# Attention, gating and experts in one program: SBUF laid out by hand, and the experts' weight loads issued at other places

## The reference

```python
# attention: B,H,S,D = 4,8,1152,64
q_pool = q.reshape(B, H, S // 2, 2, D).mean(axis=3)
attn = softmax(q_pool @ k.T / sqrt(D))          # 576 x 1152 per head
x = (attn @ v)                                  # -> tokens: 2304 x 512
# soft mixture: 8 experts, 4 slots each
logits = x @ phi                                # 2304 x 32
slot_input = softmax(logits, axis=0).T @ x      # 32 x 512
for e in range(8):                              # w1: 512 x 1024, w2: 1024 x 512
    slot_out[e] = relu(slot_input[e] @ w1[e]) @ w2[e]
x = softmax(logits, axis=1) @ slot_out          # 2304 x 512
# MLP
h = x @ w_in                                    # 512 x 2048
out = (h - tanh(h)) @ w_out                     # 2048 x 512
```

## Time and profile before

| | us |
|---|---|
| median of 3 runs | 968.81 |
| the three runs | 969.33, 964.74, 968.81 |
| the profiled execution: its own time | 964.63 |
| the profiled execution: span from the first to the last instruction | 962.8 |

### The profile page before, as it was taken

How to read it: one execution, slowest core, us unless ns; L and a number is a source line. 1 busy time by engine, 2 the same in 40 slices (tenths; PEclk the granted TensorE clock), 3 DMA queues, 4 the chain that set the end, 5 groups by cost and what they waited for, 6 DMA issues and landing times. The chain is left out here.

```text
span 962.8 us, 16386 instructions
## 1 busy us (share of the span) xinstructions
PE 887.5 (92%) x5707; PEld 641.9 (67%) x5707; DVE 588.3 (61%) x1167; ACT 496.8 (52%) x711; POOL 313.6 (33%) x215
## 2 busy tenths in 40 slices
PE   3999999999999999999999998877568999999998
PEld 2776776776776776767767765553223788888886
DVE  3676676776766766776776765450004766666663
ACT  1655555555555555555555554221006766666662
POOL 3353244244235234234333300000005744444442
PEclk9999999999999999999999999988888999999999
DMA  4322202102112022022022000295995000000000
GB/s 123 105 61 75 73 4 74 52 22 74 36 37 74 11 63 74 0 74 74 0 74 74 1 25 1 91 347 226 398 406 193 12 23 22 22 22 22 22 22 33
DMA packets 48865, 75.50 MB, mean 78 GB/s; under 512 B 5056, under 2 KB 23488, under 8 KB 48320
## 3 DMA queue, kind: packets, MB, share of 16 engines
q1 hardware_dynamic: 48832, 75.06, 22.8%
HBM read 70.32 MB, written 4.72 MB: 78 GB/s over the span
## 5 line engine op out<-in xcount | busy, mean ns | idle before, releaser
L496 DVE TENSOR_REDUCE part_neg<-ps 128x1 f32<-128x512 f32 (+1 forms) x432 | 220.9, 548 | 7.0 <-PE ps L304 6.6
L320 PE MATMUL ps<-ident,prob 128*128 128x128 f32 x1296 | 205.3, 286 | 18.4 <-ACT prob L542 7.9
L320 PEld LDWEIGHTS ps<-ident,prob 128*128 128x128 f32 x1296 | 143.9, 141 | 105.2 <-DVE probT L415 38.7
L415 DVE COPY probT<-ps 128x512 f32<-128x512 f32 (+1 forms) x256 | 125.1, 489 | 143.4 <-PE ps L320 117.1
L542 ACT ACTIVATE prob<-ps,neg_max 128x1152 f32<-128x1152 f32 x144 | 175.6, 1219 | 58.7 <-DVE neg_max L500 58.2
L304 PE MATMUL ps<-kT,qT_hi 128*128 128x512 f32 (+1 forms) x480 | 176.3, 384 | 5.3 <-DVE qT_lo L205 5.2
L553 ACT ACTIVATE probT<-ps 128x512 f32<-128x512 f32 x144 | 86.2, 598 | 171.9 <-PE ps L320 170.1
L337 PE MATMUL ps<-probT,v_nat 128*64 128x256 f32 (+1 forms) x1152 | 167.5, 417 | 0.5 <-DVE probT L415 0.5
L304 PE MATMUL ps<-kT,qT_lo 128*128 128x512 f32 (+1 forms) x480 | 159.5, 356 | 0.0
L304 PEld LDWEIGHTS ps<-kT,qT_hi 128*128 128x128 f32 x480 | 95.4, 201 | 21.6 <-issue 11.2
L1005 PE MATMUL ps<-w_hi,g 128*128 128x512 f32 x320 | 102.6, 392 | 2.2 <-POOL g L1090 2.0
(11 more groups left out here) (146 smaller groups left out, 1093.2 us busy)
## 6 DMA issues: line engine op xcount, KB each, us to landing
ring<-in_moe_w SPq DMA_DIRECT2D x10, 2048.0 KB, 20.0
k_nat<-in_k SPq DMA_DIRECT2D x16, 576.0 KB, 4.0
v_nat<-in_v SPq DMA_DIRECT2D x16, 576.0 KB, 5.1
q_nat<-in_q SPq DMA_DIRECT2D x32, 256.0 KB, 4.5
w_first<-in_moe_w SPq DMA_DIRECT2D x4, 2048.0 KB, 13.9
out<-x SPq DMA_DIRECT2D x18, 256.0 KB, 2.0
x<-in_moe_w SPq DMA_DIRECT2D x2, 2048.0 KB, 11.4
x<-in_moe_w_in SPq DMA_DIRECT2D x1, 4096.0 KB, 29.5
```

Source lines behind the costliest of these rows:

```text
L320: last = nc.tensor.transpose(block_at(s, kt), src[:, kt * P:(kt + 1) * P], ident[:])
L415: return eng_copy(probT[g][:, k0:k1, h, col:col + P], src.rearrange("p (c q) -> p c q", c=n))
L496: nc.vector.reduce_max(part_neg[:, c:c + 1], slot_banks(s)[:, c, 0:(CHUNK[c][1] - CHUNK[c][0]) * P], AX.X, negate=True).then_inc(part_done, 1)
```

## The change

The tiles get fixed addresses from a table in place of the stacked allocations. The ring of five places becomes ten halves of 2 MB (16 KB per partition), `slot` 0 to 9; expert e uses halves 2(e mod 5) and 2(e mod 5) + 1. Halves 0 and 1 overlap no other tile. Halves 2 and 3 lie over the attention's k_nat, k_parts, q_nat, q_dup and q_raw, half 4 over kT and qT of the even pairs, half 5 over those of the odd pairs, half 6 over part of probT0, halves 7 and 8 over x, half 9 over the rest of probT0 and part of probT1, where the gating has xT and c_parts. Each expert has a semaphore for each of its matrices. What SP issues, and after what:

| where | before | now |
|---|---|---|
| pair 0 | w1[0] | w1[0], w2[0] |
| pair 15, ahead of its v | | w1[1], w2[1], after the last transposes and split of q and k |
| pair 15, behind its v | | w1[2], after pair 14's last scores |
| end of attention | | w2[2] after the last scores; w1[3] after the first half of the last pair's products with v |
| gating | w2[0], w1[1], w2[1], w1[2], w2[2], at once | w2[3], w1[4] after the slot inputs (L694 of before); w2[4] after L707 of before |
| experts | w1[3], w2[3], w1[4], w2[4] at once; then experts 5 to 7, w_in, w_out by `w_used` | experts 5 to 7, w_in (two DMAs), w_out by `w_used` |

POOL zeroes `hz` at the start of the gating instead of at the start of the experts. The scratch tiles of the MLP lie at other places of the same sizes. No arithmetic changes.

```diff
@@ attention, SP @@
             def body(p, par, first, last):
                 if not last:
                     load_prep(p + 1)
+                if last:
+                    sp.wait_ge(ktr_full, PAIRS * 2)
+                    sp.wait_ge(qtr_full, PAIRS)
+                    sp.wait_ge(q_low, PAIRS)
+                    prefetch(sp, 0)
                 wait(sp, pv_done, p * 2 - 2)
                 sp.dma_start(v_nat[par][:].rearrange("p h t d -> p h (t d)"), v_src[:, bass.ds(p * 2, 2), :]).then_inc(v_in[par], 16)
+                if last:
+                    sp.wait_ge(scores_full, p * TILES * NCH)
+                    prefetch(sp, 1)
                 wait(sp, exp_done, p * TILES + TILE.index(MIX) + 1)
...
             over_pairs(sp, body)
+            sp.wait_ge(scores_full, PAIRS * TILES * NCH)
+            prefetch(sp, 2)
+            sp.wait_ge(pv_done, PAIRS * 2 - 1)
+            prefetch(sp, 3)
@@ gating @@
         def _(sp):
-            load_weights(sp)
+            sp.wait_ge(s4_full, 1)
+            load_weights(sp, 0)
+            sp.wait_ge(c_full, 1)
+            load_weights(sp, 1)
+
+        @block.gpsimd
+        def _(pool):
+            nc.gpsimd.memset(hz[:], 0.0).then_inc(hz_zero, 1)
...
             last.then_inc(s4_full, 1)
+            pe.wait_ge(hz_zero, 1)
             pe.wait_ge(s4_evac, 1)
@@ experts @@
-            pe.wait_ge(hz_zero, 1)
             up(0)
...
-            pe.wait_ge(w1_in[use[0]], use[1])
+            pe.wait_ge(win_in, 32)
...
-            nc.gpsimd.memset(hz[:], 0.0).then_inc(hz_zero, 1)
             nc.gpsimd.memset(edge[:], -SMALL * SMALL / 3.0).then_inc(consts, 1)
@@ program @@
+    SLOTS = [AT, AT + HALF * 4, AT + 2 * HALF * 4, AT + 3 * HALF * 4, ODD, EVEN, PT, NEVER["x"], NEVER["x"] + HALF * 4, PT + HALF * 4]
...
         def early(sp):
             sp.dma_start(phi[:], dram["moe_phi"].rearrange("(k p) s -> p k s", p=P)).then_inc(phi_in, 16)
-            load(sp, 0, (0,))
+            load(sp, 0, 0)
+            load(sp, 0, 1)
+
+        def prefetch(sp, n):
+            for e, part in (((1, 0), (1, 1)), ((2, 0),), ((2, 1),), ((3, 0),))[n]:
+                load(sp, e, part)
+
+        def between(sp, n):
+            for e, part in (((3, 1), (4, 0)), ((4, 1),))[n]:
+                load(sp, e, part)
+
+        def late(sp, w_used):
+            for e in range(RING, E):
+                sp.wait_ge(w_used, e - RING + 1)
+                load(sp, e, 0)
+                load(sp, e, 1)
+            sp.wait_ge(w_used, 4)
+            src = dram["moe2_w_in"].rearrange("(k p) f -> p k f", p=P)
+            for n in range(2):
+                sp.dma_start(win[n].rearrange("p (k f) -> p k f", k=KD // 2), src[:, n * KD // 2:(n + 1) * KD // 2, :]).then_inc(win_in, 16)
```

More of the change, by code:

```diff
@@ L12, with attention @@
 BANK = 512
-def attention(nc, dram, sizes, x, ident, rep, rep_ready, rep_step, early):
+def attention(nc, dram, sizes, sb, x, ident, rep, rep_ready, rep_step, early, prefetch):
     B, H, S, D = sizes
@@ L832, in experts_mlp @@
         hid = [sb(f"hid{i}", [P, FG]) for i in range(2)]
-        hz = sb("hz", [P, E, HALF, CG, NS])
         so4 = sb("so4", [P, DM])
@@ L1155, in program, with rows @@
     KD = DM // P
-    SLOT = KD * FE + (FE // P) * DM
-    RING = 5
+    HALF = KD * FE
+    BASE = (nc.sbuf_base + 31) // 32 * 32
+    def rows(start, *items):
+        table = {}
+        for name, size in items:
+            table[name] = start
+            start += size * 4
+        return table
+    KV, QT, QR = S // P, SQ // P, SQ % P
+    QC = 2 * QT * P + 3 * QR
+    XW = B * H // 2 * (QT + 1) * P
+    G0W, G1W = KV * 2 * (2 * P + QR), KV * 2 * 2 * P
+    NT, LW = B * (QT + 1), B * P + QR
@@ new lines, in program @@
+    PT = ATTENTION["probT0"]
+    SLOTS = [AT, AT + HALF * 4, AT + 2 * HALF * 4, AT + 3 * HALF * 4, ODD, EVEN, PT, NEVER["x"], NEVER["x"] + HALF * 4, PT + HALF * 4]
+    END = PT + 2 * HALF * 4
+    KEPT = rows(TOP, ("c4T", B * SQ), ("u4", FF), ("col", 8), ("line", 128), ("unit", 8), ("row", 4 * NT), ("edge", 8), ("stand", 8))
+    GATING = {
+        **rows(SLOTS[9], ("xT0", KD * SQ), ("xT1", KD * SQ)), **rows(SLOTS[9], ("c_parts", 4 * NT * NS), ("si4", DM)),
+        **rows(END + 2048, ("hz", E * (FE // P) * NS), ("lT", LW), ("dT", LW)),
+        "l_nat": ODD + HALF * 4, "d_nat": EVEN + HALF * 4,
+    }
@@ L1158, in program @@
+    EXPERTS = {**rows(END, ("soT", KD * P)), **rows(GATING["lT"], ("hid0", FE * NS // P), ("hid1", FE * NS // P)), "so4": GATING["dT"]}
+    TABLE = {**NEVER, **ATTENTION, **KEPT, **GATING, **EXPERTS}
+    assert KEPT["stand"] + 32 <= PT and GATING["xT1"] + KD * SQ * 4 <= END + 2048
+    assert max(GATING["dT"] + LW * 4, ATTENTION["row_inv"] + 64) <= nc.sbuf_usable_end - BASE
     with ExitStack() as outer:
         def sb(name, shape, dt=F32):
-            return outer.enter_context(nc.sbuf_tensor(name, shape, dt))
@@ new lines, in program, with fp32r @@
+        attention(nc, dram, sizes, sb, x, ident, rep, rep_ready, NS, early, prefetch)
+        c4T, u4 = sb("c4T", [P, B, SQ], F32R), sb("u4", [P, FF], F32R)
+        hz = sb("hz", [P, E, FE // P // (P // NS), P // NS, NS])
+        gating(nc, sizes, sb, x, ident, rep, phi, phi_in, between, siT, c4T, hz)
+        def fp32r(name, *slots):
+            return [half(f"{name}{n}", n, F32R) for n in slots]
+        res = nc.alloc_sbuf_tensor_at("res", [P, 2 * DM], F32, offset=BASE + NEVER["x"] + 2 * HALF * 4)[:]
@@ L1240 @@
+        places = (fp32r("w_hi", 0, 1), (slot[8], slot[9]), fp32r("w_lo", 8, 9), (fp32r("g_even", 2, 3), fp32r("g_odd", 6, 7)),
+                  (slot[4], slot[5]), res)
+        experts_mlp(nc, (E, DM, FE, NS, FF, B * SQ), sb, ident, rep, siT, [(space[e], (e, 16)) for e in range(E)], (w1_in, w2_in),
+                    late, u4, (win, win_in), places, c4T[:].rearrange("p b c -> p (b c)"), dram["moe2_w_out"], out, hz)
 NAMES = ("q", "k", "v", "moe_phi", "moe_w1", "moe_w2", "moe2_w_in", "moe2_w_out")
```

129 lines of the change are left out of this document (51 added, 78 removed).

## The result

The changed kernel takes **952.25 us**, the median of four runs (950.96 to 953.65), against 966.77 us for the kernel before in the same session (964.25 to 969.33): 0.9855 of its time, interval 0.9831 to 0.9879. The profiled execution took 952.31 us, its span is 950.5 us against 962.8.

The account below looks back on a forecast made before the run. A full DMA queue up to w_in's landing was taken as the bound. Stream 7.0 us earlier plus 5.3 for one load fewer made 12.3: span 962.8 to 950.5, median 968.81 to 956.5 us, range 949.5 to 962.5.

Parts of the forecast that it names:

- The mechanism and the sum: Load stream to w_in: 7.0 us earlier start and one load fewer (5.3), so w_in 12.3 earlier and span 950.5.
- The term of one load: Stream ahead of w_in: 11 loads in place of 12, since expert 3's w1 loads in the attention, 5.3 us less.
- The tail: From w_in to the end: nothing changes, and the first products with w_in stay slow at 1.2 GHz.
- rival B: First products with w_in: the clock stays up, 2.8 us better, 953.7, given a shorter PE idle time; chance 0.06.
- as before: At w_in: soT ready at 708.8, w_in in place at 712.7, so w_in late by 3.9 us, unchanged.
- The scale: From span to median: the usual run taken as the upper one, 968.81 - 12.3 = 956.5 us; the profiled execution's like 952.3.
- The queue does not run dry: DMA queue ahead of w1[5]: released 3.1 us ahead of the queue's end; gap taken as nothing, bounds 0 to 3.2 us.
- The hz memset is not a second gain: Zeroing hz in the gating: PE starts experts 1.8 us earlier but waits at w_in anyway; no gain, no cost.
- A: Rival: small stalls at w1[5]'s queue gap, pair 1's q and the gating's start give back 3 to 6 us; chance 0.14.
- C: Rival: gating loads don't start the stream early, SP or queue still held; only 5.3 us remain, 963.5; chance 0.05.
- D: Rival: instruction fetches in the last two pairs wait behind the weights, two costing 21 us, 977.5; chance 0.04.

Follow-up runs that it names:

- e1: Changed kernel with the loads back at the places of the kernel before, keeping the new layout and early hz: 964.53 us, 1.0003 of the kernel before.
- e2: Changed kernel with w2[3], w1[4] and w2[4] issued at the experts' start instead of in the gating: 959.58 us, 0.9941 of the kernel before.
- e3: Changed kernel with w1[3] issued in the gating ahead of w2[3] instead of in the attention: 957.85 us, 0.9909 of the kernel before.
- e6: Changed kernel with all attention loads but w1[0] moved to the gating's start: 953.54 us, 0.9869 of the kernel before.
- e5: Changed kernel with expert 5's weights waiting for down(1) instead of down(0): 957.65 us, 0.9915 of the kernel before.
- e4: Changed kernel with hz zeroed at the experts' start, as in the kernel before: 955.96 us, 0.9892 of the kernel before.
- e9: Changed kernel with hz zeroed at the experts' start, the same as e4 run again: 956.17 us, 0.9901 of the kernel before.
- e10: Changed kernel with w_in loaded in halves by columns and spare transposes in the gating's waits: 948.7 us, 0.9817 of the kernel before.
- e8: The changed kernel run again, nothing altered, in a later session on another chip: 952.89 us, 0.9863 of the kernel before.
- e11: e10 with 28 more spare transposes ahead of up(6) and of up(7): 950.29 us, 0.9825 of the kernel before.

## Why the prediction was right, and where it was off

**The mechanism and the sum held.** SP's issue of w2[3] was put at 651.6 and came at 651.55; w1[5] at 667.5, and it came at 666.63; there is no hole near 670. e1, e2, e3 and e6 show that the earlier start and the missing load are the gain up to w_in: neither the layout nor the attention's loads carry any of it. That the span came out at the forecast's 950.5 to a tenth is luck, since two pairs of errors cancel. The gating began 0.55 us earlier than in the profile of before, but the 40 products that end with `s4_full` took 6.70 us in place of 6.24. And w_in was 0.9 later than forecast, but what follows it 0.9 shorter, as the next two paragraphs say.

**The term of one load came out smaller.** 5.3 us were charged, and L is 4.4 shorter (4.6 by e3). So w_in was in place at 713.59 and not at 712.7, and `up(7)` began at 698.29 and not at 697.4. The working divided four loads by four, two of each kind, and took the mean for the one kind that was removed; by the rates seen that explains 0.3 us. The rest stays open: e1 against e2 gives 5.3, just what was charged.

**The tail was 0.9 shorter**, and cancels this. The first eight products with w_in take 5.44 us and not 6.36, because the clock is back at 2.4 GHz sooner. That is a third of rival B. But B's condition was wrong: it asked for a shorter idle time of PE ahead of w_in, and that time is longer now, 6.23 us against some 4.7 (from 720.5 to 725.17). Over the runs these eight products took anything from 5.20 (e2) to 6.61 (e5). The 3.9 us by which w_in was to be late "as before" became 713.59 - 708.13 = 5.5 for the same reason as the longer idle time: PE went from `up(7)` to soT complete in 9.8 us in place of 11.4, with `up(7)` itself at 1.93 us in place of 3.34.

**The scale was the larger miss.** The profiled execution's like would be 952.3, and it took 952.31; I added 4.2 us because two of the three runs shown of before were of the upper group. Over all sessions 30 of its 47 runs lie between 963.4 and 965.4 and 17 between 967.0 and 969.7. The low group was the usual one, and its scale would have given 952.3 for a median of 952.25. For the same reason the ratio of 0.9855 flatters the change a little: two of the four runs of before in that session were of the upper group and none of the changed kernel's. Low group against low group, the gain is the 12.3 us of the two profiles, 1.3%.

**"The queue does not run dry" held, narrowly.** The estimate of 3.1 us ahead of the queue's end, against about 3.2 for its start and end, was read as no gap; the edge found by e4 to e6 and e9 is at R of about 16.5, and the kernel is 1.4 us this side of it. Both marks were misplaced by about the same: the release is 15.1 behind S and not 15.9, because the first 64 products of the experts took 5.35 us and not 6.22, and the queue's end, by e5, 18.0 and not 19.0. **"The hz memset is not a second gain" was half right.** Alone it is none (e1). Together with the early stream it moves w1[5] away from that edge, which the text used in its own release time (the 1.81 us taken off 669.34) without counting it as the memset's worth: 0.2 us by e9's profile, 2.3 by e4 against e6. In the gating it cost nothing: 1.80 us on POOL, while DVE's memset beside it took 0.17 us and PE's wait ahead of its first transposes 1.02, both as before. The Trainium skill ("SBUF — State Buffer", section "SBUF: two separate sides") has GpSimd and some VectorE operations lock shared ports for a whole instruction; by that up to 1.8 us could have been lost here, and these two rows show no such loss.

**The rivals.** A: none of its three stalls came. At pair 1 POOL's q_dup began at 57.11, where 57.7 was forecast, and PE's transposes at 63.00 without a wait; L212 waits 1.42 us for ACT where 1.5 was expected to remain. C fell with S at 651.55. D fell as well: packets of code came in 560 to 618 us beside the loads, three on queue q8 and three on q14, and in the attention there the longest wait of the kind "issue" of PE's weight loads is 0.6 us, as before; the gating didn't start later.

## What to carry to other kernels

Where the end is set by a full DMA queue, as here, its start, its bytes and its holes count, and not where the earlier loads stand: move the start to the first moment at which a region is free, take out whole loads that can land earlier, and leave the rest where it is simple. Write down for each load that waits for a consumer how far its issue is ahead of the queue's end, since a shift of 2 us there turned a free delay into one paid one for one. Then look at what the waiting engine needs first: splitting w_in along the dimension that PE walks gave 4.0 us of span between two profiles for a few lines, beside 12.3 for the whole change. The runs show that gain only together with the filled gating (e10).

## What the runs showed of the hardware

**The clock falls at different moments in executions of one program.** e8 is the changed kernel itself. Up to 618.0 us its profile and the earlier one agree within 0.1 us, with the same idle time of 1.02 us ahead of the gating's first transposes; then its clock falls to 1.2 GHz. The window of e8, and that of the changed kernel's first profile:

```profile
620.00:624.00 4.00, 4.00 (x17) 2.65 (x16) 1.26 (x2) 0.89 (x2) 0.00 (x0) 0.50 0.00 0
```

```profile
620.00:624.00 4.00, 3.84 (x24) 2.51 (x23) 1.88 (x3) 1.48 (x3) 0.00 (x0) 1.00 0.00 0
```

PE does 17 products there in place of 24, and all that follows is later: S is at 655.74 in place of 651.55, 4.2 us. The profiled execution took 956.38 us, and e8's other runs are 951.45 to 953.81 and one more 956.46. So a fall there puts an execution of the changed kernel into the upper group; e11's profile has it too. It isn't the only one. In e3 the clock fell for a part of these transposes (7.97 us in place of 6.75), in e4, e5 and e6 at 654 to 660 us (5.25 to 5.37 us in place of 3.20 for the 20 transposes), which cost e6 little and, by the late release of w1[5], e4 and e5 much more. That such falls also make the upper group of the kernel before is likely, as its groups are as far apart, but no profile fell into it. What decides whether the clock falls, no run shows.

**SP is held in an issue** when three loads of 2 MB are under way: 0.38, 0.58 and 0.51 us for the first three, 8.73 for the fourth (e6). A load that is to be issued on time must not stand behind a full queue.
